# A new order of TensorE's, ScalarE's and VectorE's steps in the attention stage of a fused kernel

## The reference

```python
# attention: q, k, v are (4, 8, 1152, 64)
q_pool = q.reshape(B, H, S // 2, 2, D).mean(axis=3)          # 576 pooled rows
scores = scale * q_pool @ k.T
attn = softmax(scores);  x = attn @ v                        # (2304, 512) after a reshape
# first feed-forward: 512 -> 2048 -> 512
h = x @ w_in;  g = where(h >= 1, h, where(h <= -1, 0, (h + 1)**2 / 4));  x = g @ w_out
# second: 512 -> 768 -> 512, three gates
h = max(x @ w1, x @ w2, x @ w3);  out = h @ w_out
```

## Time and profile before

| | us |
|---|---|
| median of three timed runs | 1243.48 |
| the profiled execution | 1244.4 |
| its span, first to last instruction | 1242.7 |
| attention stage (TensorE) | 0 to 532 |
| feed-forward stages | 532 to 1242 |

### The profile page before, as it was taken

How to read it: one execution, slowest core, us unless ns; L and a number is a source line. 1 busy time by engine, 2 the same in 40 slices (tenths; PEclk the granted TensorE clock), 3 DMA queues, 4 the chain that set the end, 5 groups by cost and what they waited for, 6 DMA issues and landing times.

```text
span 1242.7 us, 19281 instructions
## 1 busy us (share of the span) xinstructions
PE 1223.2 (98%) x7061; PEld 1074.9 (87%) x7061; DVE 732.5 (59%) x1508; ACT 618.2 (50%) x1433; POOL 274.7 (22%) x240
## 2 busy tenths in 40 slices
PE   7999999999999999999999999999999999999998
PEld 6999999999999999878888888888898878787887
DVE  5999999999999999853443443443452132212222
ACT  5898899889988998832222222222331111112011
POOL 3133333333333333379000000000192000000000
PEclk8999999999999999999999999999999999999999
DMA  3565656666666664434100000000041010101010
GB/s 95 96 114 114 116 115 116 116 115 116 116 115 115 113 116 79 78 98 143 30 1 1 1 1 1 1 1 1 2 136 33 1 34 1 35 1 35 1 35 17
DMA packets 124604, 76.17 MB, mean 61 GB/s; under 512 B 62560, under 2 KB 111712, under 8 KB 124512
## 3 DMA queue, kind: packets, MB, share of 16 engines
q1 hardware_dynamic: 124512, 74.94, 29.8%
HBM read 47.71 MB, written 4.79 MB: 42 GB/s over the span
## 4 chain that ended last, share of the span: by engine, by line
PE 94%; DVE 2%; ACT 2%; issue 0%; SPq 0%; DMA 0%; POOL 0%; DVEq 0%; ACTq 0%
PE hid L936 34%; PE acc L962 16%; PE values L519 12%; PE trans L437 11%; PE scores L502 7%; PE scores L503 6%; PE acc L994 5%; PE trans L457 1%; PE trans L447 1%; DVE neg_max_parts L649 1%; DVE pT_lo L663 1%; ACT probs L568 1%; ACT qT L1027 0%; ACT pT_hi L559 0%; DVE qT L1033 0%
## 5 line engine op out<-in xcount | busy, mean ns | idle before, releaser
L936 PE MATMUL hid<-qT,w_slots 128*128 128x512 f32 (+1 forms) x1680 | 367.8, 372 | 0.0
L936 PEld LDWEIGHTS hid<-qT,w_slots 128*128 128x128 f32 x1680 | 293.6, 188 | 61.2
L649 DVE TENSOR_REDUCE neg_max_parts<-scores 128x1 f32<-128x384 f32 x432 | 227.1, 550 | 8.9 <-PE scores L503 4.3
L663 DVE TENSOR_TENSOR pT_lo<-trans,pT_hi 128x384 fp32r<-128x384 f32 x432 | 225.7, 546 | 5.0 <-ACT pT_hi L559 4.4
L559 ACT ACTIVATE pT_hi<-trans 128x384 fp32r<-128x384 f32 x432 | 205.8, 494 | 42.0 <-PE trans L437 38.8
L568 ACT ACTIVATE probs<-scores,neg_max 128x768 f32<-128x768 f32 (+1 forms) x288 | 212.5, 742 | 6.5 <-DVE neg_max L656 5.6
L437 PE MATMUL trans<-ident,probs 128*128 128x128 f32 x1296 | 201.0, 275 | 4.9 <-DVE pT_lo L663 2.8
L502 PE MATMUL scores<-kT,qT 128*128 128x384 f32 x480 | 182.4, 380 | 2.0 <-ACT probs L568 1.5
L437 PEld LDWEIGHTS trans<-ident,probs 128*128 128x128 f32 x1296 | 155.9, 140 | 20.5 <-DVE pT_lo L663 8.9
L503 PE MATMUL scores<-kT,qT 128*128 128x384 f32 x480 | 162.6, 339 | 0.0
L1059 ACT ACTIVATE excess<-rise,halves 128x512 f32<-128x512 f32 (+1 forms) x80 | 54.5, 681 | 185.9 <-DVE rise L1129 185.9
(11 more groups left out here) (77 smaller groups left out, 1494.2 us busy)
## 6 DMA issues: line engine op xcount, KB each, us to landing
kT<-k_split SPq DMA_DIRECT2D x60, 288.0 KB, 5.4
k_raw<-in_k SPq DMA_DIRECT2D x32, 288.0 KB, 6.1
v_raw<-in_v SPq DMA_DIRECT2D x32, 288.0 KB
q_raw<-in_q SPq DMA_DIRECT2D x32, 256.0 KB, 3.2
k_split<-value_all SPq DMA_DIRECT2D x64, 72.0 KB, 2.9
out<-X SPq DMA_DIRECT2D x18, 256.0 KB, 2.9
q_raw<-in_moe_w_out SPq DMA_DIRECT2D x14, 256.0 KB, 3.1
k_raw<-in_moe_w SPq DMA_DIRECT2D x12, 256.0 KB, 3.2
```

Source lines behind the costliest of these rows:

```text
L649: dve.tensor_reduce(neg_max_parts[:, par, n:n + 1], scores[:, score_banks(s)[n], 0:SB], AX_X, ALU.max, negate=True).then_inc(parts_done, 1)
L663: dve.tensor_tensor(*tile_places(pT[1], src, s % TILES, g), hi.bitcast(F32), ALU.subtract).then_inc(p_lo_done, 1)
L936: last = pe.matmul(out_bank, weight(slot, part, half, k), x[:, k, cols], start=(k == 0 and part == 0 and x is x_hi), stop=(k == KC - 1 and ...
```

## The change

The three tables are written anew. No other line is touched, and each table names the same steps. On TensorE, K0 goes from the third place to behind `T0.1`, K1 from the end of tile 0 to the end of tile 2; K2, which stood between `S4.2` and `S4.0`, follows K1 behind `S4.0`; `S2.0` goes ahead of `T0.0`, `T2.2` ahead of `S4.0`, `Q2` from tile 6 to tile 5, and the value products are cut at other places. ScalarE's and VectorE's lists follow; `R` is VectorE's first step.

```diff
 PE_ORDER = """
-S1.2 S1.0 K0
-T0.0 W2:10-14 S2.0 T0.1 W2:14-16 T0.2 S2.1 W2:16-18 S2.2 K1 S3.0 W3:0-9
-T1.0 S3.1 S3.2 T1.1 W3:9-10 T1.2 W3:10-12 S4.1 W3:12-13
-T2.0 T2.1 S4.2 K2 S4.0 T2.2
-T3.0 W3:13-17 S5.0 T3.1 W3:17-18 T3.2 S5.1 S5.2 Q0 V0:0-2
-T4.0 S6.0 V0:2-8 T4.1 V0:8-9 Q1 S6.1 S6.2 T4.2
-T5.0 V0:9-18 S7.1 T5.1 S7.2 T5.2 S7.0 S8.0
-T6.0 V1:0-9 Q2 V1:9-11 T6.1 S8.1 S8.2 T6.2
-T7.0 V1:11-18 T7.1 S9.0 T7.2 S9.1 S9.2
-T8.0 T8.1 V2:0-2 S10.1 V2:2-9 T8.2 V2:9-10
+S1.2 S1.0 S2.0
+T0.0 W2:10-13 T0.1 W2:13-16 K0 W2:16-18 S2.1 S2.2 T0.2 W3:0-8 S3.0
+T1.0 W3:8-9 S3.1 S3.2 T1.1 T1.2 W3:9-12 S4.1 W3:12-13
+T2.0 T2.1 S4.2 T2.2 S4.0 K1 K2 W3:13-16 S5.0 W3:16-17
+T3.0 W3:17-18 T3.1 T3.2 S5.1 S5.2 S6.0 Q0 V0:0-6
+T4.0 V0:6-8 T4.1 V0:8-9 S6.1 S6.2 Q1 T4.2 V0:9-15 S7.1
+T5.0 V0:15-17 S7.2 Q2 T5.1 V0:17-18 S7.0 S8.0 T5.2 V1:0-6
+T6.0 T6.1 V1:6-9 S8.1 S8.2 T6.2
+T7.0 V1:9-12 S9.0 V1:12-15 T7.1 V1:15-17 T7.2 V1:17-18 S9.1 S9.2
+T8.0 T8.1 V2:0-3 S10.1 V2:3-9 T8.2 V2:9-10
 """
 ACT_ORDER = """
-K0
-H0.0 E1.0 E1.1 H0.1 W2 H0.2 K1 E2.0 E2.1
-H1.0 H1.1 H1.2 E3.0
-H2.0 E3.1 H2.1 K2 H2.2
-H3.0 E4.0 H3.1 W3 E4.1 H3.2 Q0
-H4.0 E5.0 H4.1 Q1 E5.1 H4.2
-H5.0 E6.0 E6.1 H5.1 V0 H5.2
-H6.0 E7.0 Q2 E7.1 H6.1 H6.2
-H7.0 E8.0 H7.1 V1 H7.2 E8.1
+H0.0 E1.0 H0.1 W2 K0 E1.1 H0.2 E2.0
+H1.0 E2.1 H1.1 H1.2 E3.0
+H2.0 E3.1 H2.1 H2.2 K1 K2 E4.0
+H3.0 E4.1 W3 H3.1 H3.2 Q0 E5.0
+H4.0 E5.1 H4.1 Q1 H4.2 E6.0
+H5.0 E6.1 H5.1 V0 Q2 H5.2 E7.0
+H6.0 E7.1 H6.1 H6.2
+H7.0 E8.0 H7.1 H7.2 V1 E8.1
 H8.0 H8.1 E9.0 E9.1 H8.2
 """
 DVE_ORDER = """
-K0 R
-L0.0 M2.0 M2.1 M2.2 L0.1 M3.0 L0.2 K1 M3.1 M3.2
-L1.0 L1.1 L1.2 M4.1
-L2.0 M4.2 L2.1 M4.0 K2 L2.2 M5.0
-L3.0 L3.1 M5.1 M5.2 L3.2 Q0
-L4.0 M6.0 L4.1 M6.1 M6.2 Q1 L4.2 M7.1
-L5.0 M7.2 M7.0 L5.1 L5.2
-L6.0 M8.0 Q2 M8.1 M8.2 L6.1 L6.2
-L7.0 M9.0 L7.1 M9.1 M9.2 L7.2 M10.1
-L8.0 L8.1 M10.2 M10.0 L8.2
+R M2.0
+L0.0 M2.1 M2.2 L0.1 K0 L0.2 M3.0 M3.1 M3.2
+L1.0 L1.1 M4.1 L1.2
+L2.0 M4.2 L2.1 M4.0 L2.2 K1 K2 M5.0
+L3.0 M5.1 M5.2 L3.1 L3.2 Q0 M6.0
+L4.0 M6.1 M6.2 L4.1 Q1 L4.2 M7.1
+L5.0 M7.2 M7.0 Q2 L5.1 M8.0 L5.2
+L6.0 M8.1 M8.2 L6.1 L6.2
+L7.0 M9.0 L7.1 M9.1 M9.2 L7.2
+L8.0 M10.1 L8.1 M10.2 M10.0 L8.2
 """
```

## The result

The changed kernel takes 1246.57 us (median of eight runs, 1244.62 to 1248.07), the kernel before 1243.44 (eight runs, 1241.06 to 1244.90): ratio 1.0026, 95% interval 1.0016 to 1.0036. It is slower by 3.1 us, a little over what a measurement can tell from no change. The forecast was 1243.0; the sign that it held to be least likely came, inside its range.

The account below looks back on a forecast made before the run. TensorE and VectorE were taken as bounds, each 30.8 of a calm pair's 31.4 us. Calm pairs 1.0, pair 0 0.3 and long pairs -1.8 gave -0.5 us, put on the median: about 1243.0 us, range 1237.5 to 1248.0.

Parts of the forecast that it names:

- the sum of the calm pair: TensorE's waits in one calm pair: 0.46 us before, 0.54 after, a rise of 0.08, 1 us in 14 pairs.
- The long pairs: Seven reciprocal intervals 0.3 to 1.7 us longer, 5.4 in all, ScalarE's H2.2 late; a third taken as gain, -1.8 us.
- Pair 0: First pair of the attention stage: VectorE idles 0.3 to 0.4 us more at M2.1, +0.3 us.
- Pair 15: Last pair of the attention stage, without K and Q: little difference, 0, give or take 0.5 us.
- A: Rival, faster: the tables take out waits and the new ones don't come up; 1236 to 1240, say 1238.0 us; chance 0.36.
- B: Rival, slower: way from S4.0 over M4.0, L2.2, K1, K2 to T3.2; 0.3 to 0.35 us a pair, 1248.0; chance 0.18.
- B2: Rival, slower: SP queue makes ScalarE's V1 keep wait for GpSimd's add; 0.3 us a pair, 1248 us; chance 0.03.
- (2): Expected mark: T3.2 waits on VectorE's K step 0.1 to 0.2 us in each pair, none at T7.1.
- (3): Expected mark: VectorE idle before M2.1 by 0.2 to 0.3 us.
- (5): Expected mark: ScalarE's V1 keep does not stand behind GpSimd's add.
- (1): Expected mark: calm intervals between VectorE's reciprocals of 31.3 to 31.6 us.
- (4): Mark to check: whether ScalarE's H2.2 is still late in some pairs and by how much the pair grows.

Follow-up runs that it names:

- the kernel with tiles 2 and 3: Old tables, K1 gone from tile 0, changed tables for tiles 2 and 3, contiguous reciprocal store, against the kernel before: 1247.46 us, 1.0013.
- its twin without the small store: Old tables, reciprocals stored as 36 contiguous bytes per partition (values wrongly scaled), against the kernel before: 1239.04 us, 0.9946.

## Why the prediction was wrong, step by step

**The frame held.** The feed-forward part did not move; a pair's own work is 30.8 us on both engines and only waits changed; the change moves the time by less than 0.3%.

**The step that failed is the sum of the calm pair**, "Before 0.46 ... 0.54", with its working in tiles 2 and 3 and tiles 4 to 8. The 0.46 was right (0.47). After it the forecast named 0.54, and the same method finds 0.82. Term by term: S3.1 0.02 against 0.12, T3.0 ("just fit (0.0)") against 0.07, S7.0 not named against 0.08, S7.2 0.07 against 0.14, S1.0 near 0 against 0.06, T4.0 0.10 against 0.13; on the other side T6.1's 0.13 did not come and T3.2 was 0.14, not 0.19. S3.1, T3.0 and S1.0 have one thing in common: by the forecast their covers fit to within 0.05 us. The distances of the forecast were right (1.04, 0.60), but a step that comes just in time loses 0.06 as a transpose and 0.05 to 0.1 as a score step, and the sheet counted it as nothing. Over 14 pairs 0.28 instead of 0.08 us is 3.9 us instead of 1.1. That is 2.8 us, where the two profiled executions missed the forecast by 2.5 (+2.0 against -0.5), so this term is the miss, and the others together gave a little back.

**K1's second role was overlooked.** Under tile 0 only K0 was priced, and the 0.02 of S3.1 in the sum has no working. The 0.33 us of K1 ahead of S3.0 was the reserve of S3.1, as the kernel with tiles 2 and 3 shows (0.28). The forecast itself asks for every cover that goes when a step is moved, and did not ask it here.

**The long pairs.** "Nothing that the trace names holds it" and "a third of 5.4": the size was near, -1.5 against -1.8, the mechanism open. They did not go; they fell on K1 and its neighbours, at the time when the store ends. Not all of them are the store's: pair 3's wait at T7.1 is in every order. Their gain of 1.5 us is no merit of the order that could be relied on: the kernel before varies from 1241 to 1252 us over the chips of this study, its twin without the small store by 1.2 us over five runs.

**Pair 0** was forecast at +0.3 and costs 0.6 at full clock (32.96 against 32.34 us): the idle time at M2.1 and a 2.2 us wait of S2.1 for E1.0 came. That the sum of the two profiled executions has -0.1 in its place is luck, of where the stretch at half clock fell. **Pair 15**: 0 forecast, -0.4 measured, inside its bound; without the small store it is +0.06, so the forecast was right for the order.

**The rivals.** A (sheet too pessimistic) fell. B was right about place and sign: T3.0, T3.2 and T4.0 behind the chain of both K steps carry 0.34 of the new 0.82 us; its condition, S4.0 later than on the sheet by 0.2, did not hold (0.05 as before). B2 did not occur: the add that V1's keep needs starts at 204.40 and the keep at 207.61. Of the five marks, (2), (3) and (5) came as written, (1) did not: 31.7 us, the bound at which the text called itself wrong, and (4) H2.2 is no longer late, K1 is. The forecast had set aside the rule of the Trainium skill on VectorE's pipe ("VectorE: DVE Perf Modes", section "The DRAIN you can't avoid"). It left out that the same paragraph excepts a next operation that is not held, which starts earlier. The changed kernel's rows are of that kind too: L2.2 and K1 start 0.46 us apart (190.98 to 191.44) where L2.2's record is 0.55 us long. So setting the rule aside was right and has no part in the miss. The count beside it was off: a pair has 60 large operations (27 L, 27 M, 3 K, 3 Q) and not 63, which at 0.55 us makes 33 us and not 35, still more than 31.4.

**The chances.** 0.22 for slower was low. At least three hand-overs (S1.0, S3.1, T3.0) were laid out to fit within 0.05 us; errors of such fits go one way, since a hand-over can lose time and not gain any. An error of 0.15 us a pair should not have been put on both sides of zero, and the miss, 0.20, was larger still.

## What to carry to other kernels

When an order is laid out by hand, give each hand-over between engines some 0.1 us of reserve, and count one that fits exactly as a loss of 0.05 to 0.1. Compare two orders by their ledger of calm periods on a base without disturbances, since a median with long pairs of chance in it hid two fifths of this change's cost. And look at the page's packet counts before the order: a store of 4.5 KB a pair in pieces of 4 bytes cost 5 to 7 us in the old order, more than the new tables moved, and one transpose on TensorE repaired it.

## What the hardware showed that I had not expected

With a store of 1152 pieces of 4 bytes under way no engine's completion signal is recorded for 0.8 to 1.2 us in half of the pairs, and with two such stores for up to 8 us. A score matmul that is released just as TensorE comes to it is followed by its second after 0.28 us instead of 0.18, without being late itself. VectorE's waits and TensorE's can be traded for each other at no change in the period, in three of three tries.
